# Woven attention units: loads of q, k and v issued by ScalarE instead of SyncE

## The reference

```python
# attention: each chunk of 32 queries sees 8 memory keys, 16 keys to its left, itself, 8 to its right
for c in range(nc):
    l_start, r_end = max(0, c_start - 16), min(S, c_end + 8)
    k_full = np.concatenate([mem_k, k[:, :, l_start:r_end]], axis=2)
    v_full = np.concatenate([mem_v, v[:, :, l_start:r_end]], axis=2)
    scores = scale * np.matmul(q_c, k_full.transpose(0, 1, 3, 2))
    a = np.exp(scores - np.max(scores, axis=-1, keepdims=True))
    a = a / (np.sum(a, axis=-1, keepdims=True) + 1e-09)
    out[:, :, c_start:c_end] = np.matmul(a, v_full)
x = attn_out.transpose(0, 2, 1, 3).reshape(3072, 512)
h = x @ w_in                      # layer 1: ELU between the two products
x = np.where(h > 0, h, np.exp(np.minimum(h, 0)) - 1) @ w_out
r = np.maximum(x @ w_in2, 0)      # layer 2: s * relu^2 + b between them
out = (s * (r * r) + b) @ w_out2
```

## Time and profile before

| what | value |
|---|---|
| time of the kernel (median of 3 runs) | 1128.06 us (1126.26 to 1129.08) |
| span of the profiled execution | 1125.1 us |
| busy: PE / ACT / DVE / POOL | 97% / 69% / 73% / 32% of the span |
| mean granted clock of TensorE | 0.995 of full speed |
| DMA | 300.71 MB, nearly all on one queue; 112760 of 203479 packets are under 512 B |

### The profile page before, as it was taken

One profiled execution on the slowest core, in us unless ns is written; L12 is line 12 of the kernel. 1 busy time (PEld: TensorE's weight loads), 2 busy tenths in 40 slices (PEclk: granted clock), 3 DMA queues, 4 the chain that ended last, 5 costly groups with the idle time before them and its releaser, 6 DMA issues.

```text
span 1125.1 us, 18153 instructions
## 1 busy us (share of the span) xinstructions
PE 1091.9 (97%) x5787; PEld 872.4 (78%) x5787; DVE 820.6 (73%) x1235; ACT 781.9 (69%) x1842; POOL 357.3 (32%) x402
## 2 busy tenths in 40 slices
PE   8998989889999999999999999999999999999998
PEld 4766767677777777788887888888888888888886
DVE  5895788368867856987968968869657578566485
ACT  4996877567677657768768677677676476774574
POOL 7588788550012432105465023771000000000000
PEclk9999989999999999999999999999999999999999
DMA  9998999999798898979899688998696666776664
GB/s 197 248 273 269 368 337 335 345 304 335 215 283 270 238 258 261 312 232 384 299 358 336 203 316 329 339 334 262 191 302 204 199 189 191 219 224 190 191 198 155
DMA packets 203479, 300.71 MB, mean 267 GB/s; under 512 B 112760, under 2 KB 120952, under 8 KB 203384
## 3 DMA queue, kind: packets, MB, share of 16 engines
q1 hardware_dynamic: 203384, 299.55, 86.8%
HBM read 224.00 MB, written 75.50 MB: 266 GB/s over the span
## 4 chain that ended last, share of the span: by engine, by line
PE 72%; ACT 5%; POOL 3%; DVE 3%; DMA 3%; issue 2%; ACTq 0%; SPq 0%; POOLq 0%; DVEq 0%
PE ps L1050 37%; PE ps L1035 31%; DMA w_ring<-w_scratch 2%; ACT ps L1135 2%; PE ps L944 1%; PE ps L996 1%; ACT elu L1228 1%; DVE g_lo L1552 1%; ACT elu L1233 1%; POOL w_new L846 1%; PE ps L969 1%; POOL att L846 1%; PE ps L938 1%; PE ps L953 1%; POOL t_more L846 1%
## 5 line engine op out<-in xcount | busy, mean ns | idle before, releaser
L1035 PE MATMUL ps<-xc_hi,w_ring 128*128 128x512 f32 x1344 | 433.9, 395 | 9.6 <-DMA w_ring<-w_scratch 4.5
L1050 PE MATMUL ps<-g_hi,w_ring 128*128 128x512 f32 x1344 | 420.7, 394 | 5.4 <-issue 3.5
L1035 PEld LDWEIGHTS ps<-xc_hi,w_ring 128*128 128x128 f32 x1344 | 252.9, 188 | 68.0 <-DMA w_ring<-w_scratch 5.4
L1050 PEld LDWEIGHTS ps<-g_hi,w_ring 128*128 128x128 f32 x1344 | 249.8, 189 | 62.9 <-issue 5.4
L1050 PE MATMUL ps<-g_lo,w_ring 128*128 128x512 f32 x672 | 262.9, 391 | 0.0
L1035 PE MATMUL ps<-xc_lo,w_ring 128*128 128x512 f32 x672 | 262.3, 390 | 0.0
L846 POOL TENSOR_TENSOR w_new<-w_raw,w_new 128x256 fp32r<-128x256 f32 x159 | 152.7, 966 | 250.7 <-ACT w_new L1285 248.3
L1552 DVE TENSOR_TENSOR g_lo<-X,g_hi 128x512 fp32r<-128x512 f32 x240 | 175.0, 735 | 22.6 <-ACT g_hi L1268 22.0
L1268 ACT ACTIVATE g_hi<-X 128x512 fp32r<-128x512 f32 x240 | 150.1, 630 | 59.3 <-PE ps L1050 56.3
L1050 PEld LDWEIGHTS ps<-g_lo,w_ring 128*128 128x128 f32 x672 | 126.7, 189 | 27.0
L1035 PEld LDWEIGHTS ps<-xc_lo,w_ring 128*128 128x128 f32 x672 | 126.7, 188 | 24.1
(11 more groups left out here) (128 smaller groups left out, 1324.9 us busy)
## 6 DMA issues: line engine op xcount, KB each, us to landing
w_ring<-w_scratch SPq DMA_DIRECT2D x332, 512.0 KB, 4.5
w_scratch<-w_new SPq DMA_DIRECT2D x159, 256.0 KB, 5.3
w_scratch<-att SPq DMA_DIRECT2D x39, 256.0 KB, 6.2
w_raw<-in_moe_w_in SPq DMA_DIRECT2D x16, 512.0 KB, 6.0
w_raw<-in_moe_w_out SPq DMA_DIRECT2D x16, 512.0 KB, 6.1
x_scratch<-y SPq DMA_DIRECT2D x12, 512.0 KB, 6.3
att<-x_scratch SPq DMA_DIRECT2D x12, 512.0 KB, 6.4
out<-elu SPq DMA_DIRECT2D x24, 256.0 KB, 4.3
```

Of the source, the lines that this page charges most:

```text
L1035: last = nc.tensor.matmul(bank_of(st, st.i), w[:, a, cols], x[:, st.pi, kk, :], start=(st.pi in (P1, P5) and kk == 0 and n == 0), stop=(kk ...
L1050: last = nc.tensor.matmul(bank_of(st, d), w[:, a, cols], x[:, k % RING, :], start=(st.pi in (P1, P5) + (P4,) * (1 - st.gr) and st.i == 0 a ...
```

## The change

The five DMA issues of each woven unit move from SP's program to ACT's; the DMAs of the first 17 units stay with SP. In SP's loop, `load_qk` of a unit stood after `load_weights(d)` with 2d = w0 + 10 of the unit before, and `load_v` with 2d = w0 + 20. In ACT's loop, they stand at the end of iteration w0 + 2 and w0 + 13 of the unit before, behind `cut_w` and `copy_qT`. For the first woven unit both stand in iteration 4. With w0 = 10 + 12c, the loads of woven unit c (counted from 0) are at g = 12c for q and k and g = 12c + 11 for v. The sizes, the destinations and the semaphores are the same.

```diff
 @block.sync
             def load_qk(n):
                 b, blk = divmod(n, UPB)
-                done = qk_first[n % AHEAD] if n < HEAD else qk_in
-                if n == HEAD:
-                    sp.wait_ge(pv_done, HEAD)
-                elif n >= AHEAD:
-                    sp.wait_ge(qT_done, n + 1 - (AHEAD if n < HEAD else 1))
-                    sp.wait_ge(kT_done, n + 1 - (AHEAD if n < HEAD else 1))
+                done = qk_first[n % AHEAD]
+                if n >= AHEAD:
+                    sp.wait_ge(qT_done, n + 1 - AHEAD)
+                    sp.wait_ge(kT_done, n + 1 - AHEAD)
...
                 for n, w0 in WOVEN:
-                    if n == HEAD and d == W_RING + 1 or n > HEAD and d == (WOVEN[n - HEAD - 1][1] + 10) // 2:
-                        load_qk(n)
-                    if n == HEAD and d == W_RING + 2 or n > HEAD and d == (WOVEN[n - HEAD - 1][1] + PV + 8) // 2:
-                        load_v(n)
                     if d == (w0 + PV + 10) // 2:
                         save_x0(n)
...
 @block.scalar
+            def load_qk(n):
+                b, blk = divmod(n, UPB)
+                act.wait_ge(pv_done, HEAD)
+                act.wait_ge(qT_done, n)
+                act.wait_ge(kT_done, n)
+                first, last = blk * QU - LEFT, blk * QU + QU + RIGHT
+                lo, hi = max(first, 0), min(last, S)
+                act.dma_start(heads(q_of(n)), rows(q, b, blk * QU, blk * QU + QU)).then_inc(qk_in, 16)
+                act.dma_start(heads(k_of(n)[lo - first:hi - first]), rows(k, b, lo, hi)).then_inc(qk_in, 16)
+                act.dma_start(heads(k_of(n)[CTX:KEYS]), rows(mem_k, b, 0, MEM)).then_inc(qk_in, 16)
+
+            def load_v(n):
+                b, blk = divmod(n, UPB)
+                act.wait_ge(pv_done, n)
+                first, last = blk * QU - LEFT, blk * QU + QU + RIGHT
+                lo, hi = max(first, 0), min(last, S)
+                act.dma_start(heads(v_of(n)[lo - first:hi - first]), rows(v, b, lo, hi)).then_inc(v_in, 16)
+                act.dma_start(heads(v_of(n)[CTX:KEYS]), rows(mem_v, b, 0, MEM)).then_inc(v_in, 16)
...
                 for n, at in woven_at(g):
                     if at == Q_T:
                         copy_qT(n)
+                for n, w0 in WOVEN:
+                    if n == HEAD and g == 4 or n > HEAD and g == WOVEN[n - HEAD - 1][1] + 2:
+                        load_qk(n)
+                    if n == HEAD and g == 4 or n > HEAD and g == WOVEN[n - HEAD - 1][1] + PV + 1:
+                        load_v(n)
```

More of the change, by code:

```diff
@@ L612, in g_raw, with heads, rows @@
             return T2[:, st.i, :] if st.pi in (P6, P4) else X[:, RAW_OF[st.pi], st.i, :]
+        def heads(ap):
+            return ap.rearrange("p (h d) -> p h d", h=H)
+        def rows(src, b, lo, hi):
+            return src[bass.ds(b, 1), :, lo:hi, :].rearrange("b h s d -> s (b h) d")
         block = ctx.enter_context(nc.Block())
@@ L641, in load_v @@
                 b, blk = divmod(n, UPB)
-                done = v_first[n % AHEAD] if n < HEAD else v_in
+                done = v_first[n % AHEAD]
                 if n >= AHEAD:
-                    sp.wait_ge(pv_done, n + 1 - (AHEAD if n < HEAD else 1))
+                    sp.wait_ge(pv_done, n + 1 - AHEAD)
                 first, last = blk * QU - LEFT, blk * QU + QU + RIGHT
```

## The result

The changed kernel took 1140.41 us in the median of 4 runs (1135.58 to 1144.09) against 1127.55 us (1126.26 to 1129.08): ratio 1.0102, 95% interval 1.0066 to 1.0138, 1% slower. A second set of runs of the same kernel (`e8_after_again`) gave 1.0109 (1.0078 to 1.0140). The profiled execution took 1138.37 us, its span is 1136.6 us.

A forecast was written before the change was run, and what follows sets the result against it. It took crowded DMA engines, and ACT in an order PE follows closely, to bound the 105 to 300 us stretch. Span 1125.1 + 12.7 (ACT) - 4.7 (SP) = 1133.1, plus 2.96: 1136 us, 0.7% slower; range 1118 to 1150.

The forecast's parts named there:

- rival (b): ACT's cost and SP's relief cancel at about 5 us each, giving 1128 us; chance 0.15.
- What lies around the span: Time outside the profiled span, added to the predicted span to give the kernel time: 2.96 us.
- What it costs on ACT, the price of an issue: Each issue assumed to hold ACT as long as SP, by medians: 3.45 us per load_qk, 0.90 per load_v.
- Step 4: First woven unit: both loads together block ACT 4.35 us, hidden at 0 us cost; about 7 us with the maxima.
- Steps 12 and 24: Second and third units: ACT has almost no slack, so the block reaches PE less 0.6 us run-ahead: 2.85 us each.
- Units 4 to 7: Steps 36 to 72: ACT's gaps of about 2 us hide most; 0.5 us each, 2 us; bounds 0 and 4 each.
- Units 8 to 15: Steps 84 to 168: ACT's blocks mostly hidden; 0.25 us each, 2 us; bounds 0 and 1.5 each.
- The fourteen `load_v`: Other load_v issues on ACT, 0.9 us each, mostly in gaps: 0.2 us each, 3 us; bounds 0 and 0.9 each.
- What it gives on SP: SP's ring loads, saves and raw loads leave earlier, shortening PE's waits: 4.7 us gained, at most 7.8, at least nothing.
- Rival (a): SP's relief, over 8 us, outweighs ACT's cost, under 4, as issues fall into ACT's gaps: 1119 us; chance 0.27.
- Where the loads start: Starting q and k 2 to 3 steps earlier, v about 1, is worth nothing; cover 8 steps, 11 us.
- Rival (c): No gain on SP and long ACT blocks, load_qk taking 6.9 us: cost 26 us, 1154 us; chance 0.15.

The follow-up runs named there:

- the tiny loads: Kernel before, plus 128-byte loads issued by ACT into a tile nobody reads, 10 and 3 at the changed kernel's two load places per woven unit: ratio 1.0220.
- e5_v_after: Changed kernel with load_v four steps later (three for the first unit), so v and mem_v queue behind the next unit's q, k and mem_k: ratio 1.0022.
- e9_mem_first: Against the kernel before: q, k and mem_k issued by ACT with mem_k first, v and mem_v left on SP: ratio 0.9955.
- e2_qk_only: Against the kernel before: only q, k and mem_k issued by ACT, v and mem_v left on SP: ratio 0.9964.
- e10_tiny_early: Kernel before, plus ten 128-byte loads issued by ACT into an unread tile at each of steps 12 and 24: ratio 1.0047.
- e12_sp_mem_first: Kernel before, all loads on SP, with mem_k issued ahead of q and k for the woven units: ratio 1.0001.
- e11_tiny_late: Kernel before, plus ten 128-byte loads issued by ACT into an unread tile at each of eight places, steps 84 to 168: ratio 1.0122.
- e1_v_only: Against the kernel before: only v and mem_v issued by ACT, q, k and mem_k left on SP: ratio 1.0015.
- e3_late_mem: Changed kernel with mem_k issued three steps later (four for the first unit), still by ACT: ratio 1.0027 to the kernel before.

## Why the prediction was right

Measured by the two medians, the change was +12.9 us; the forecast was +8 us, with the sign and the mechanism for it: ACT's blocks cost PE more than SP's relief gave. That a block on ACT alone costs PE time is shown by the tiny loads.

**What was luck.** The size, and with it how clearly the sign shows, came of something that the prediction doesn't hold. The same 75 issues on ACT, with v not one step ahead of q and k (`e5_v_after`), cost 0.22% (0.03 to 0.40), nearer to rival (b), which had 0.15, than to the forecast of 0.7%. The q, k and mem_k issues of the changed kernel take 49.0 us in all, close to 15 x 3.45 = 51.8, but only because a few are long: in the mean they were as said, in the median much shorter.

**What lies around the span.** The sum added 2.96 us. In the runs that give both figures it is 1.7 to 1.8 us (1138.37 and 1136.6 for the changed kernel), so 1.2 us of the forecast had no such source.

**What it costs on ACT, the price of an issue.** I took the medians of SP, 3.45 us for `load_qk` and 0.90 for `load_v`. By the median ACT's are lower (0.325 + 0.564 + 1.330 = 2.2 us and 0.82 us), and what matters is not the median but the six units of 4.0 us and more. I had seen that mem_k takes longest and supposed that it waits for room behind q and k. `e9_mem_first` shows it right that the wait comes from standing behind them, and `e5_v_after` that v, one step ahead of all three, makes more long ones: six in the changed kernel, four when it was run again, one in `e5_v_after`, two in `e2_qk_only`. That the order of the issues decides was no step of mine.

**Step 4.** Said 4.35 us and hidden. ACT was held from 101.20 to 106.78; PE waited 0.82 us for the s2 copy at 107.58. Within the bounds.

**Steps 12 and 24.** Said 2.85 us each, with waits on seeds and on the probabilities. The waits came as named (2.8 us together and 3.35 us); by the marks 1.6 and 1.1 us of loss, by `e10_tiny_early` 2.7 us for each block of 5.2 to 5.4. The rule "the block passes to PE whole but for 0.6 us" was too strict: about half passes.

**Units 4 to 7.** Said 2 us, bounds 0 and 4 each. Against `e12_sp_mem_first` the marks say 3.4 + 2.2 + 4.8 us for steps 36 to 60, 10.4 us, and 3.9 + 0.0 + 5.3 in `e8_after_again`; step 72 shows none. This is where the sum was most wrong. The largest losses are step 60, a k of 2.41 and a mem_k of 4.38 us and then a wait of 3.75 us for s3, and step 36, a 5.12 us issue and then three waits on low parts, with the fall of the clock behind them. So a lower clock did follow the new stalls, as the prediction had allowed for, but only once and for 1.7 us. I had taken the gaps before each place for slack, but a gap in which ACT waits for PE is over as soon as PE is through; only what PE can do without ACT is slack.

**Units 8 to 15.** Said 2 us. The marks say 1.6 + 0.2 + 1.7 = 3.5 us at steps 96 to 120 and none elsewhere, since the other blocks lasted 1.4 to 2.1 us. With longer blocks the same places cost 1.7 us each (`e11_tiny_late`). The slack I read there was right for short blocks and much too large for those over 4 us.

**The fourteen `load_v`.** Said 3 us. `e1_v_only`: 1.0015, 1.7 us within an interval that holds none. As a direct cost this fits, as far as that interval goes. Their indirect cost, through mem_k of the next unit, is the larger part of the change: the step from 1.0022 to 1.0109, 10 us.

**What it gives on SP.** Said 4.7 us, at most 7.8. The ring waits did go, and so did the wait for s3 at 111.57. In the five traces with q and k on SP that show them, the two waits that recur make 4.6 to 5.4 us, so the term was of the right size. Rival (a), relief over 8 us and ACT's cost under 4, is what `e9_mem_first` comes near to (-5 us). The gain with q and k on ACT can't be the time that SP is held, since `e12_sp_mem_first` frees SP of 32 us for no gain. The two differ clearly: on the same chip `e9_mem_first` took 1122.89 us and `e12_sp_mem_first` 1126.91, in the median of 12 runs each. Where the gain lies is shown by PE's waits above, the one for s3 behind the mark of step 10 and the one on the ring behind that of step 70. Ahead of the first, ACT's `cut_w` into `att` stands still, 2.74 us in the kernel before and 4.02 in `e12_sp_mem_first`, and holds the s3 copy behind it. What remains as its cause is where q and k lie: on SP they are ahead of the saves and ring loads in the same queue. That step is argued, not shown: the ring's median landing was 7.4 us in `e9_mem_first` and 6.1 in `e12_sp_mem_first`, the other way round.

**Where the loads start.** Said nothing, with a cover of 8 steps, 11 us. The changed kernel shows no wait for its loads. But the first unit has only the six steps from 4 to 10, 8.3 us by the earlier trace rows, and there `e9_mem_first` waited 3.18 us for k.

The Trainium skill, "DMA: Bandwidth & Descriptors", section "Issuing engines are not separate DMA queues", says that issuing from several engines only saves sequencer time. In bytes moved the traces agree (the DMA share between 105 and 410 us is 0.98 in the kernel before and 0.99 with q and k on ACT). But saving sequencer time on SP was worth nothing within its interval and moving the q, k and mem_k issues was worth 0.4%, so the rule doesn't cover what happened here.

**Rival (c)** had blocks of 6.9 us in every unit. They came, 7.2 us at worst, but in few. The Trainium skill, "Perfetto Trace Analysis", section "DMA Instruction — HWDGE (DVE, Sync)", has the issuing sequencer stay with its instruction until all its descriptors are made, and wait for a lock first. The first fits the long issues. For the second, the trace shows SP starting and ending four issues inside ACT's issue of 5.12 us at step 36, so ACT's long issue did not shut SP out; whether short waits for each other occur no run singled out.

## What to carry to other kernels

Before a DMA issue is moved to a compute engine, read how long each issue holds its queue, at its worst and not in the median, and ask what the engine next in line may be late by; here blocks of up to 2 us were free and of those over 4 us PE paid a third to two thirds. And compare traces with more than one execution of the kernel before: a single one put the largest loss at the wrong step. The order within a queue sets that time: put small loads with few rows ahead of large ones (this shortened the issues, from 32.5 to 19.6 us on ACT; that it shortens the kernel was not shown), and do not issue a large load just before the others (this was worth 0.9%). And when two parts of a change are timed alone, time them together too: here 0.9964 and 1.0015 made 1.010.

## What was unexpected

A load of 16 KB in eight rows held ACT for up to 5.0 us behind two loads of 192 and 240 KB (median 0.59), and ahead of them for 0.28 us in the median and 0.60 at most (`e2_qk_only` and `e9_mem_first`); on SP the medians were 2.09 and 0.47 us. In place of mem_k, k did not become long; with v one step ahead it did, 4.84 us at step 60 in `e3_late_mem`. A load of 128 bytes, issued in a row with others, held ACT for 442 ns in the median, more than q with its 192 KB (325 ns).
